# Top-32 attention with a gated product: weight splits evenly over stages 0 to 8, the sign of tile 1 on ScalarE from the first unit, the keys' low part later on GpSimd

## The chip, the cores and the metric

One core of a Trainium2 chip. The metric is the device time of one execution in microseconds, the median of three runs; the profile is of one further execution, whose own time is given beside its span.

## What is computed

```python
scores = scale * np.matmul(q, k.transpose(0, 1, 3, 2))       # q, k, v: 4 x 8 heads x 576 x 64
kth = np.partition(scores, -32, axis=-1)[..., -32:-31]
scores = np.where(scores >= kth, scores, -1e9)
attn = exp(scores - max) / (sum + 1e-9)
x = (attn @ v) as 2304 tokens x 512
out = ((x @ w_a) * (x @ w_b)) @ w_out                        # w_a, w_b: 512 x 1536, w_out: 1536 x 512
```

All is float32. The kernel multiplies in a faster format (fp32r) and keeps the accuracy by splitting each operand into a high part, which is the number rounded to that format, and a low part, which is what is left; each product is high x high + high x low + low x high.

## The kernel before, in words

A **unit** is a tile of 128 query rows for a pair of heads; there are 72, and a unit holds two tiles of scores (j = 0 and 1, one a head), 128 x 576 each. The order of units runs over the four batches. In **stage** s each engine does its share of a software pipeline whose order is written out by hand, in five loops over s from 0 to 78, one an engine; engines meet only in semaphores.

- VectorE works on unit s: four rounds of MAX8 (`find`) with MATCH_REPLACE8 between them (`take_out`), which give the 32 largest of each row; the inverse of unit s - 1's sums (`invert`) between the second round and the third; and at the end `below` (L1008), one compare a tile, which writes a large negative number to `keep` wherever a score is under the 32nd. From unit SIGN0 = 10 on only tile 0 has a compare. For tile 1 ScalarE computes the sign of (score - 32nd) into the top byte of `keep` (`mask_sign`, L715), over a fill value that VectorE's memset put there once.
- GpSimd, stage s: `negate(s-1)` (L882), which waits for VectorE's unit s - 1; the two masking adds `masked` (L901); `split_k`, the low part of keys that were prepared in stage s - 1 (L866); `hidden_lo`, the low part of a*b (L917); weight splits 2, 3, 4 of stage s - 1 (L856); `hidden`, the product a*b (L908); the low parts of x (L893) and q (L874); weight splits 0 and 1 of stage s.
- ScalarE, stage s: both exponentials of unit s - 1 (L724), `guard` (L732), split 0, `x_out`, the copy of b (L773), scores of the first half of unit s + 1 (L702), split 1, `normalise` of tile 0 (L739), scores of the second half, split 2, `normalise` of tile 1, the copies of the transposed probabilities (L747, L749), `mask_sign(s)`, `copy_q(s+3)`, split 3, the hidden copies (L780, L782), the copy of a, prepared keys, split 4.
- TensorE, stage s: probabilities times v of unit s - 2 (L557), scores of unit s + 1 (L523), the first product x @ w_a of chunk n = s - 5 (L588), turning a*b (L599), transposing the probabilities of unit s - 1 (L539), which waits for `normalise`, q's transposes (L501), the output product of chunk n - 2 (L620), and x @ w_b of chunk n.
- SP issues nearly all DMAs, in the same order of stages, and waits in it.

**Weights.** The 36 blocks of 128 x 512 come through a ring of four tiles `stage`. Block i is loaded by SP once the low part of block i - 4 is made; ScalarE rounds it into `w_hi` (L662); GpSimd subtracts (L856) into `w_lo`, or, for the 18 blocks whose low parts don't stay in SBUF (those of w_out and of w_b's last two row blocks, k 2 and 3), into one of LOWS buffers in the last slot of the ring of keys, from where SP stores it to scratch memory (L398) and reloads it per chunk. A low buffer is written again only when its store has landed. `W_ORDER` is the order of blocks, `W_AT` gives the (stage, place) of each split, with the places 0 to 4 named above; `columns_of` and `output` on TensorE wait for as many low parts as their first use needs. The order before is, for each third of the columns, eight blocks of w_a and w_b and then blocks of w_out (3, 3 and 6). `copy_k` of the slot that the low buffers share waits for all stores.

Of the kernel before, what the change touches and what calls it, by code (L numbers as in the profile page):

```python
# [6 lines left out]
def topk_attention_gated_product(nc, q, k, v, w_parts, xs, out):  # L7
# [8 lines left out]
    NEG = -3.0e38  # L16
# [4 lines left out]
    NF = DFF // P  # L21
# [6 lines left out]
    PAIR = 2 * S  # L28
# [8 lines left out]
    HB = HC // P  # L37
    NH = DFF // HC
    NCH = GROUPS * NH
# [50 lines left out]
    def preps_at(s):  # L90
        return [n for n in range(NPREPS) if PREP_SLOT[n] == s]


    SIGN0 = 10

    V_AT = {max(0, p - 1): [(0, p)] for p in range(1, KB)}
    V_AT[0] = [(0, 0), (0, 1)]
# [16 lines left out]
    for cb in range(NCB):  # L114
        W_BASE.append(len(W_ORDER))
        W_ORDER += [WB0 + kb * NCB + cb for kb in range(LKB, KB)] + [kb * NCB + cb for kb in range(KB)]
        W_ORDER += [WB0 + kb * NCB + cb for kb in range(LKB)]
        last = NF if cb == NCB - 1 else (cb + 1) * HB
        W_ORDER += [WO0 + f for f in range(cb * HB, last)]
    STAGES = 4  # L120
    W_AT = [(0, 2), (0, 4)] + [(1, m) for m in (0, 1, 2, 4)] + [(s, m) for s in range(2, 5) for m in range(5)]
    W_AT += [(s, m) for s in range(5, 9) for m in (0, 1, 2, 4)]
    W_AT = W_AT[:WCH]
    LOWS = 2
    LAST_IN_AB = NCH - NH - 1
    LATE_WO = (NCH - 4, NCH - 3, NCH - 2)
    LATE_WB = (NCH - 3, NCH - 1)

    def w_of(s, m):
        return [W_AT.index((s, m))] if (s, m) in W_AT else []  # L130


    LEAVING = [i for i in range(WCH) if W_ORDER[i] >= LOW]
# [5 lines left out]
    with ExitStack() as ctx:  # L139
# [37 lines left out]


        keys = k_t[:].rearrange("p k i c -> p (k i c)")
        leaving = keys[:, (KPAIRS - 1) * PAIR:(KPAIRS - 1) * PAIR + LOWS * WC].rearrange("p (n c) -> p n c", n=LOWS)  # L180

# [124 lines left out]
        def unit(u):  # L308
            return 0 <= u < NU
# [347 lines left out]
        def _(act):  # L657
# [6 lines left out]
            def weights(s, m):  # L664
                for i in w_of(s, m):
                    split_hi(i)

            def copy_k(n):
                act.wait_ge(kt_done, n + 1)
                if n >= KB - 1:  # L670
                    act.wait_ge(qt_done, min(PREP_SLOT[n] + 4, NU))
                if n >= KPAIRS:
                    wait(act, qk_done, 2 * last_unit((n - KPAIRS) // KB, (n - KPAIRS) % KB) + 2)
                elif n == KPAIRS - 1:
                    for m in range(LOWS):
                        act.wait_ge(st_w[m], 16 * len(range(m, len(LEAVING), LOWS)))
                for frm, a, z in keys_in_psum(n):
                    A.copy(k_t[:, n % KPAIRS, 0, a:z], frm[:, 0:z - a]).then_inc(khi_ready, 1)
                if n > 0:
                    wait(act, klo_ready, n - 1)  # L680
                    for frm, a, z in keys_in_psum(n):
                        last = A.copy(k_whole[:, a:z], frm[:, 0:z - a])  # L682
                    last.then_inc(k_copied, 1)
# [22 lines left out]
                A.copy(scores[:, 0, j, :].rearrange("p (a c) -> p a c", a=2), ps[:, j:j + 3:2, 0:HALF]).then_inc(s_ready, 1)  # L706

            def mask_sign(u):
                if not unit(u) or u < SIGN0:
                    return  # L710
                act.wait_ge(neg_ready, u + 1)
                if u == SIGN0:
                    act.wait_ge(s_keep, 1)
                act.wait_ge(mask_done, 2 * (u - 1) + 2)
                A.activation(keep_sign, scores[:, u % ROWS, 1, 0:S], ACT.Sign, bias=neg[:, u % 2, 1, 1:2], scale=SCALE  # L715
                             ).then_inc(keep_ready[1], 1)

# [86 lines left out]
            for s in range(FIRST, MOE_END):  # L804
# [18 lines left out]
                weights(s, 1)  # L823
                normalise(s - 1, 0)
                copy_scores(s + 1, 1)
                weights(s, 2)
                normalise(s - 1, 1)
                copy_probs_t(s - 1, 0)
                copy_probs_t(s - 1, 1)
                mask_sign(s)  # L830
                copy_q(s + 3)
                weights(s, 3)
                copy_hidden(n - 1)
# [2 lines left out]
                for m in preps_at(s):  # L836
                    copy_k(m)
                weights(s, 4)
                if s == NU + 1:
                    copy_y(n - 2)  # L840
            copy_y(NCH - 1)
# [2 lines left out]
        def _(pool):  # L844
# [81 lines left out]
            for s in range(FIRST, MOE_END):  # L926
                n = s - MOE0
                negate(s - 1)
                masked(s - 1, 0)
                masked(s - 1, 1)  # L930
                for m in preps_at(s - 1):
                    if m >= KB - 1:
                        split_k(m)
                if s < NU + 2 or n >= NCH:
                    hidden_lo(n - 2)
                for m in range(2, 5):
                    weights(s - 1, m)
                hidden(n - 1)
                low_of_x(s - 2)
                if s >= NU + 2 and n < NCH:  # L940
                    hidden_lo(n - 2)
                split_q(s + 2)
                weights(s, 0)
                weights(s, 1)

        @block.vector
        def _(dve):
# [15 lines left out]
            for h in range(2):  # L963
                rows = slice((1 - h) * TAIL, (2 - h) * TAIL)
                ins = V.memset(v_rows[rows, :, TAILS, h * D:(h + 1) * D], 0.0)
            ins.then_inc(s_vpad, 1)

            def find(u, r):
                nonlocal count
# [42 lines left out]
            for s in range(NU):  # L1012
# [11 lines left out]
                take_out(s, 2, 1)  # L1024
                find(s, 3)
                below(s, 0)
                if s < SIGN0:
                    below(s, 1)
                elif s == SIGN0:
                    dve.wait_ge(mask_done, 2 * s)  # L1030
                    V.memset(keep[:, 1, :], NEG).then_inc(s_keep, 1)
            invert(NU - 1)

# [28 lines left out]
```

## Time and profile before

| | us |
|---|---|
| median of 3 runs | 818.16 (817.97 to 818.72) |
| the profiled execution's own time | 817.8 |
| its span | 815.4 |
| PE, DVE, ACT, POOL busy | 771.7, 744.3, 657.0, 507.4 |
| granted TensorE clock, mean | 0.98 |

Lines with an L are lines of the kernel before. A timeline row is start, length, engine, line, operation, output<-inputs, shapes and count, and in brackets how long the engine stood idle before it and what ended that. Length of "x2" rows is that of both together. A wait row is: who waited, for whom, in total, how many times, the longest. All times are microseconds from the span's start.

### The profile page before, as it was taken

The numbers are of one execution on the slowest core, as the hardware profiler recorded it, in microseconds if no ns is written. First come the engines' busy times: TensorE is split into PE (matmuls) and PEld (weight loads), VectorE is DVE, ScalarE is ACT, GpSimd is POOL, SyncE is SP. The second block draws the span as 40 slices with busy tenths as digits, with TensorE's granted clock in tenths as the row PEclk, the third lists the DMA queues.
The fourth block names the chain that finished last, engine by engine and source line by source line (L and its number), as shares of the span: only waits on it lengthen the run. The fifth ranks groups of instructions, "written<-read, shape, count | busy, mean of one in ns | idle before, by whom it ended". The sixth has DMA issues, their size and how long they took to land.

```text
span 815.4 us, 18431 instructions
## 1 busy us (share of the span) xinstructions
PE 771.7 (95%) x5952; PEld 686.3 (84%) x5952; DVE 744.3 (91%) x1603; ACT 657.0 (81%) x1614; POOL 507.4 (62%) x560
## 2 busy tenths in 40 slices
PE   5368899999999999999999999999999999999998
PEld 4246788899998989898889899989998889898887
DVE  6999999998999999999999999999999999999500
ACT  5678978888888888888888888888888888888732
POOL 2989986656555666666756565665656555665532
PEclk9957999999999999999999999999999999999999
DMA  6566754445553444444644443544463434343562
GB/s 169 150 186 199 217 185 148 138 137 150 149 167 113 140 125 129 126 138 142 178 142 134 128 137 122 145 136 136 137 183 123 137 124 137 124 133 117 167 214 84
DMA packets 117245, 119.16 MB, mean 146 GB/s; under 512 B 61856, under 2 KB 80288, under 8 KB 117152
## 3 DMA queue, kind: packets, MB, share of 16 engines
q1 hardware_dynamic: 116880, 117.93, 47.8%
q8 instruction: 50, 0.82, 0.4%
q14 instruction: 43, 0.35, 0.2%
q10 hardware_dynamic: 272, 0.07, 0.0%
HBM read 108.53 MB, written 9.44 MB: 145 GB/s over the span
## 4 chain that ended last, share of the span: by engine, by line
PE 86%; POOL 5%; DVE 4%; DMA 2%; issue 2%; ACT 1%; SPq 0%; POOLq 0%; ACTq 0%
PE ps L588 37%; PE ps L620 18%; PE ps L557 10%; PE ps L523 9%; PE ps L539 8%; PE ps L599 3%; DVE best L976 2%; DVE work L993 2%; POOL scores L901 2%; POOL w_lo L856 1%; POOL k_t L856 1%; DMA x_scratch<-k_t 1%; PE ps L492 1%; PE ps L501 1%; DMA stage<-in_w 0%
## 5 line engine op out<-in xcount | busy, mean ns | idle before, releaser
L976 DVE MAX8 best<-work 128x8 f32<-128x576 f32 x432 | 304.4, 747 | 0.0
L901 POOL TENSOR_TENSOR scores<-scores,keep 128x576 f32<-128x576 f32 x144 | 207.0, 1441 | 37.4 <-ACT keep L715 36.6
L993 DVE MATCH_REPLACE8 work<-best,work 128x576 f32<-128x576 f32 x288 | 212.0, 745 | 0.0
L588 PE MATMUL ps<-w_hi,x_hi 128*128 128x384 f32 x576 | 202.5, 351 | 2.4 <-issue 1.2
L588 PE MATMUL ps<-w_hi,x_lo 128*128 128x384 f32 x576 | 194.4, 338 | 0.0
L908 POOL TENSOR_TENSOR ab<-ab 128x384 f32<-128x384 f32 x72 | 73.3, 1018 | 158.6 <-ACT ab L773 158.6
L588 PE MATMUL ps<-w_lo,x_hi 128*128 128x384 f32 x432 | 145.8, 337 | 0.0
L747 ACT COPY probs_t<-ps 128x512 f32<-128x512 f32 x144 | 82.2, 586 | 51.8 <-PE ps L539 49.7
L588 PEld LDWEIGHTS ps<-w_hi,x_hi 128*128 128x128 f32 x576 | 108.1, 188 | 17.5 <-issue 13.9
L724 ACT ACTIVATE scores<-scores,neg 128x576 f32<-128x576 f32 x144 | 114.4, 822 | 6.6 <-POOL scores L901 6.4
L739 ACT ACTIVATE scores<-scores,inverse 128x576 f32<-128x576 f32 x144 | 115.4, 803 | 0.3 <-DVE inverse L1003 0.3
L539 PE MATMUL ps<-ident,scores 128*128 128x128 f32 x648 | 90.1, 283 | 26.2 <-ACT scores L702 19.2
L588 PEld LDWEIGHTS ps<-w_hi,x_lo 128*128 128x128 f32 x576 | 108.1, 188 | 0.0
L993 DVE MATCH_REPLACE8 work<-best,scores 128x576 f32<-128x576 f32 x144 | 106.0, 745 | 0.0
L976 DVE MAX8 best<-scores 128x8 f32<-128x576 f32 x144 | 101.9, 750 | 2.5 <-ACT scores L706 2.5
L539 PEld LDWEIGHTS ps<-ident,scores 128*128 128x128 f32 x648 | 74.7, 145 | 33.5 <-ACT scores L739 17.8
L557 PE MATMUL ps<-probs_t,v_rows 128*64 128x128 f32 (+1 forms) x1600 | 99.5, 274 | 2.5 <-ACT probs_t L749 2.5
L557 PEld LDWEIGHTS ps<-probs_t,v_rows 128*64 128x64 f32 x1600 | 82.3, 141 | 21.0 <-issue 16.9
L702 ACT COPY scores<-ps 128x576 f32<-128x576 f32 x142 | 93.4, 658 | 2.0 <-PE ps L523 1.9
L620 PE MATMUL ps<-w_hi,h_hi 128*128 128x512 f32 x216 | 91.1, 422 | 0.5 <-issue 0.4
L523 PE MATMUL ps<-k_t,q_t 64*128 64x288 f32 x960 | 87.6, 319 | 3.3 <-ACT k_whole L682 1.9
L588 PEld LDWEIGHTS ps<-w_lo,x_hi 128*128 128x128 f32 x432 | 81.3, 188 | 3.0
(64 smaller groups left out, 1300.9 us busy)
## 6 DMA issues: line engine op xcount, KB each, us to landing
wo_lo<-x_scratch SPq DMA_DIRECT2D x69, 768.0 KB, 4.5
wb_lo<-x_scratch SPq DMA_DIRECT2D x70, 384.0 KB, 4.1
stage<-in_w SPq DMA_DIRECT2D x36, 256.0 KB, 3.1
x_scratch<-k_t SPq DMA_DIRECT2D x18, 256.0 KB, 2.4
k_rows<-in_k SPq DMA_DIRECT2D x32, 128.0 KB, 4.7
v_rows<-in_v SPq DMA_DIRECT2D x32, 128.0 KB, 2.6
out<-stage SPq DMA_DIRECT2D x16, 256.0 KB, 4.2
q_rows<-in_q SPq DMA_DIRECT2D x63, 64.0 KB, 3.5
```

Source lines behind the costliest of these rows:

```text
L523: last = mm(ps_s[half][:, j, :], q_t[rows, u % 2, qpart, first:first + 2 * D], k_t[rows, (b * KB + p) % KPAIRS, kpart, at:at + HALF], star ...
L539: last = tr(to, row_of(u)[:, at:at + P], ident[:])
L557: last = mm(ps_x[h * D:(h + 1) * D, i * w:(i + 1) * w], v_rows[:, p, block, h * D:(h + 1) * D], probs_t[:, at:at + w], start=(i == 0 and c ...
L588: last = mm(ps_ab[which], x[:, g % 2, kb, :], w, start=(kb == 0 and m == 0), stop=(kb == KB - 1 and m == 2))
L620: last = mm(ps_y, x[:, cols], w, start=(f + b == 0 and m == 0), stop=(f + b == NF - 1 and m == 2))
L702: A.copy(scores[:, u % ROWS, :, half * HALF:(half + 1) * HALF], ps_s[half]).then_inc(s_ready, 1)
L724: A.activation(row, row, ACT.Exp, bias=neg[:, u % 2, j, 0:1], scale=SCALE, accum_out=sums[:, u % 2, j:j + 1]).then_inc(e_ready, 1)
L739: A.mul(row, row, inverse[:, u % 2, j:j + 1]).then_inc(p_ready, 1)
L747: A.copy(probs_t[:, a:a + FULL * P], ps[:, 2 + j, :]).then_inc(pt_ready, 1)
L901: V.tensor_tensor(row, row, keep[:, j, :], ALU.add).then_inc(mask_done, 1)
L976: ins = V.max(best[:, u % 2, j, 8 * r:8 * r + 8], src)
L993: V.match_replace(out=work[:, j, :], in_to_replace=best[:, u % 2, j, 8 * r:8 * r + 8], in_values=src, imm_value=NEG).then_inc(chain, 1)
```

## The change

It does three things:

1. Weights: all blocks of w_out come last in `W_ORDER`. `W_AT` has four splits a stage in stages 0 to 2, five in 3 to 5, three in 6 to 8 (before: 2, 4, 5, 5, 5, 4, 4, 4, 3). There are four low buffers (LOWS) in place of two, over the last two slots of the ring of keys, so the wait for all stores stands at the preparation of the fifth pair of keys (n = 4, stage 10) instead of the sixth (stage 12).
2. `mask_sign` runs for all units. In stages 0 and 1 it stands at the end of ScalarE's stage, from stage 2 on behind the copies of the transposed probabilities. VectorE's second compare is gone, its memset of the fill value stands before its first unit.
3. On ScalarE `normalise` of tile 1 stands before weight split 2 instead of behind it; on GpSimd `split_k` stands behind `hidden_lo`.

```diff
-    SIGN0 = 10
+    SIGN_LATE = 1
...
-        last = NF if cb == NCB - 1 else (cb + 1) * HB
-        W_ORDER += [WO0 + f for f in range(cb * HB, last)]
+    W_ORDER += [WO0 + f for f in range(NF)]
     STAGES = 4
-    W_AT = [(0, 2), (0, 4)] + [(1, m) for m in (0, 1, 2, 4)] + [(s, m) for s in range(2, 5) for m in range(5)]
-    W_AT += [(s, m) for s in range(5, 9) for m in (0, 1, 2, 4)]
-    W_AT = W_AT[:WCH]
-    LOWS = 2
+    W_AT = [(s, m) for s in range(3) for m in (0, 1, 2, 4)] + [(s, m) for s in range(3, 6) for m in range(5)]
+    W_AT += [(s, m) for s in range(6, 9) for m in (0, 1, 2)]
+    LOWS = 4
...
-        leaving = keys[:, (KPAIRS - 1) * PAIR:(KPAIRS - 1) * PAIR + LOWS * WC].rearrange("p (n c) -> p n c", n=LOWS)
+        leaving = keys[:, (KPAIRS - 2) * PAIR:(KPAIRS - 2) * PAIR + LOWS * WC].rearrange("p (n c) -> p n c", n=LOWS)
...
-                elif n == KPAIRS - 1:
+                elif n == KPAIRS - 2:
...
             def mask_sign(u):
-                if not unit(u) or u < SIGN0:
+                if not unit(u):
                     return
                 act.wait_ge(neg_ready, u + 1)
-                if u == SIGN0:
+                if u == 0:
                     act.wait_ge(s_keep, 1)
-                act.wait_ge(mask_done, 2 * (u - 1) + 2)
+                wait(act, mask_done, 2 * (u - 1) + 2)
...
                 copy_scores(s + 1, 1)
+                normalise(s - 1, 1)
                 weights(s, 2)
-                normalise(s - 1, 1)
                 copy_probs_t(s - 1, 0)
                 copy_probs_t(s - 1, 1)
-                mask_sign(s)
+                if s > SIGN_LATE:
+                    mask_sign(s)
...
                 weights(s, 4)
+                if s <= SIGN_LATE:
+                    mask_sign(s)
...
                 masked(s - 1, 1)
+                if s < NU + 2 or n >= NCH:
+                    hidden_lo(n - 2)
                 for m in preps_at(s - 1):
                     if m >= KB - 1:
                         split_k(m)
-                if s < NU + 2 or n >= NCH:
-                    hidden_lo(n - 2)
...
             ins.then_inc(s_vpad, 1)
+            V.memset(keep[:, 1, :], NEG).then_inc(s_keep, 1)
...
                 below(s, 0)
-                if s < SIGN0:
-                    below(s, 1)
-                elif s == SIGN0:
-                    dve.wait_ge(mask_done, 2 * s)
-                    V.memset(keep[:, 1, :], NEG).then_inc(s_keep, 1)
```

## Rows read from the trace of the kernel before

**Rows 1.** The page: busy time by engine; busy tenths of GpSimd, slices of 20.4 us.

```profile
PE 771.7 (95%) x5952; PEld 686.3 (84%) x5952; DVE 744.3 (91%) x1603; ACT 657.0 (81%) x1614; POOL 507.4 (62%) x560
...
POOL 2989986656555666666756565665656555665532
```

**Rows 2.** Waits, 108 to 765 us: who, for whom, total us, times, longest.

```profile
DVE inverse L1003 <- ACT sums_eps L732: 14.2, 15, 1.8
...
PE ps L539 <- ACT scores L739: 1.4, 1, 1.4
```

**Rows 3.** The chain that ended last, 0 to 125 us: start, length, what.

```profile
102.42 0.34 SPq L398
...
102.80 3.56 DMA stage<-in_w
...
106.91 0.78 ACT scores L739
```

**Rows 4.** Timeline of ScalarE, 9 to 112 us, then 443 to 466 us.

```profile
57.68 0.20 ACT L732 ACTIVATE sums_eps<-sums 128x2 f32<-128x2 f32 x1
...
60.57 0.62 ACT L662 CAST w_hi<-stage 128x512 fp32r<-128x512 f32 x1 [1.30 <-DMA stage<-in_w]
...
65.48 0.27 ACT L749 COPY probs_t<-ps 128x128 f32<-128x128 f32 x1
...
68.68 0.20 ACT L732 ACTIVATE sums_eps<-sums 128x2 f32<-128x2 f32 x1
...
106.38 0.62 ACT L662 CAST w_hi<-stage 128x512 fp32r<-128x512 f32 x1 [1.00 <-DMA stage<-in_w]
...
444.73 0.97 ACT L715 ACTIVATE keep<-scores,neg 128x576 int8<-128x576 f32 x1
```

**Rows 5.** Timeline of TensorE, 60 to 125 us.

```profile
86.28 0.41 PE L588 MATMUL ps<-w_hi,x_hi 128*128 128x384 f32 x1 [0.78 <-issue]
...
95.93 0.76 PE L539 MATMUL ps<-ident,scores 128*128 128x128 f32 x5 [1.44 <-ACT scores L739]
...
107.73 0.77 PE L539 MATMUL ps<-ident,scores 128*128 128x128 f32 x5 [1.42 <-ACT scores L739]
...
112.73 1.31 PE L557 MATMUL ps<-probs_t,v_rows 128*64 128x128 f32 x20
```

**Rows 6.** Timeline of VectorE, 0 to 120 us, then 443 to 466 us.

```profile
10.29 1.42 DVE L976 MAX8 best<-scores 128x8 f32<-128x576 f32 x2 [2.48 <-ACT scores L706]
...
51.63 0.94 DVE L1008 TENSOR_SCALAR keep<-scores,best 128x576 f32<-128x576 f32 x2
...
62.19 1.97 DVE L1008 TENSOR_SCALAR keep<-scores,best 128x576 f32<-128x576 f32 x2
...
97.41 1.41 DVE L976 MAX8 best<-scores 128x8 f32<-128x576 f32 x2
...
443.87 1.43 DVE L976 MAX8 best<-scores 128x8 f32<-128x576 f32 x2
...
449.42 0.17 DVE L1003 RECIPROCAL inverse<-sums_eps 128x2 f32<-128x2 f32 x1
...
454.00 1.43 DVE L976 MAX8 best<-scores 128x8 f32<-128x576 f32 x2
```

**Rows 7.** Timeline of GpSimd, 70 to 125 us, then 443 to 466 us.

```profile
96.70 0.44 POOL L882 TENSOR_SCALAR neg<-best 128x4 f32<-128x4 f32 x1
...
101.12 2.51 POOL L856 TENSOR_TENSOR k_t<-stage,w_hi 128x512 fp32r<-128x512 f32 x2
...
443.64 0.41 POOL L882 TENSOR_SCALAR neg<-best 128x4 f32<-128x4 f32 x1 [1.33 <-DVE best L976]
```

**Rows 8.** Line 856: what GpSimd idled for before it, us and times.

```profile
  DMA x_scratch<-k_t: 3.0, 5
```

**Rows 9.** Windows: length, busy PE, PEld, DVE, ACT, POOL, PEclk, DMA, GB/s.

```profile
65.00:70.00 5.00, 4.37 (x34) 3.59 (x33) 5.00 (x13) 4.97 (x15) 5.00 (x5) 0.50 0.33 97
70.00:75.00 5.00, 3.27 (x20) 2.74 (x21) 5.00 (x9) 3.85 (x7) 4.13 (x6) 0.98 0.86 267
```

More of the change, by code:

```diff
@@ L129, in w_of @@
     def w_of(s, m):
-        return [W_AT.index((s, m))] if (s, m) in W_AT else []
+        return [i for i in range(WCH) if W_AT[i] == (s, m)]
     LEAVING = [i for i in range(WCH) if W_ORDER[i] >= LOW]
```

## The prediction

> **What bounds the kernel now.** I read the page first: TensorE is busy 771.7 us of 815.4 and VectorE 744.3, so either could set the end [rows 1]. Next, who waited from 108 to 765 us: TensorE for another engine only once, 1.4 us, and that is the wait that ends at 107.73, the beginning of this stretch [rows 2]. After 107.73 the end is therefore TensorE's own work in a fixed order, which the change leaves alone, and VectorE's waits there, 14.2 us in 15 times [rows 2], cost nothing. So the kernel is 107.7 us of filling and about 708 us of TensorE with hardly a pause; the change is worth what it moves TensorE's last wait.
>
> The chain of waits up to there [rows 3]: SP stores a low part at 102.42 and behind that loads the next block, 3.56 us. ScalarE has stood 1.00 us at this split and takes it at 106.38 [rows 4]; only then does it scale tile 1 of unit 7 (106.91, done 107.68 by 0.77 of work). TensorE has waited 1.42 us for that, and 1.44 us for the same thing a stage earlier, at 95.93 [rows 5]. From 107.73 it has 5.0 us to the product with v that opens its next stage at 112.73 [rows 5].
>
> Beneath this lies VectorE's pace. I call start(s) the time at which it begins unit s: start(0) = 10.29, start(8) = 97.41, so a unit takes 10.89 in the mean; in the steady part 454.00 - 443.87 = 10.13 [rows 6]. Two things make the difference. Units 0 to 9 have a second compare (L1008). And where GpSimd is busy at a unit's end the pair of compares takes 1.97 us in place of 0.94 [rows 6]; so it is in three of the eight units, and in a fourth by half.
>
> The sum needs start(8) and the distance from it to the end of the last scaling of unit 7.
>
> **Part 1: sign of tile 1 on ScalarE from unit 0.** Ten compares go, and one sign comes in each of units 0 to 9: 0.97 us on ScalarE, as later on [rows 4]. The fill value's memset (a pass over one tile, about half of the pair's 0.94) moves ahead of VectorE's first search, where it idles 2.48 for scores [rows 6]: nothing. Eight units at 10.13 from 10.29 put start(8) at 91.3, against 97.41.
>
> That is too good by the port. In units 4 to 7 the one remaining compare still finds GpSimd in a run of subtractions, 2.51 for two [rows 7]. The bounds are 0 (all slip in between two) and 1.0 each, as 1.97 - 0.94; I take the half, 0.5 x 4 = **2.0**, bounds 0 to 4.0. The Trainium skill (SBUF — State Buffer, "SBUF: two separate sides") has VectorE and GpSimd hold a shared port pair as an exclusive lock for a whole instruction. The trace agrees (1.97 for 0.94); by that rule every compare that comes second pays the rest of a subtraction; with all four paying 1.0 the time would be 2.0 us later than mine.
>
> The new wait: GpSimd's second masking add now waits for ScalarE. Queued behind it on GpSimd are the weight splits, the product a*b and the low parts of x and q, for which SP's next loads and ScalarE's next splits wait. The sign itself stands, from unit 2 on, behind the copies of the transposed probabilities of the unit before; behind it come copy_q, splits 3 and 4, the hidden copies and both exponentials. That closes a loop. From the end of one guard (57.88) to the last of those copies (65.75) it is 7.9 us now, 1.30 of it a wait for a weight at 60.57; from there to the next guard's end (68.88) 3.1 [rows 4]; with the sign between, 0.85 of ScalarE's time as it overlaps its neighbour, 11.9 in all, over 10.13. Part 3 takes one split, 0.5, off the first piece; of the 1.30 I keep 0.9 in stages 4 and 5, which have five splits still, and 0 from stage 6 on. So some 11.2 there (a little more with the copy of a), 10.4 after. VectorE's play: the inverse stands 5.55 us into a unit (449.42 - 443.87, [rows 6]); a guard that nothing delays ends 4.4 into it (negation 0.23 before the start and 0.41 long, two adds 2.9, exponential and guard 1.2), so 1.1 us. Walked with these pieces: guard 3 ends at 56.1, needed at 50.8 + 5.55 = 56.4, just in time. Stage 4: 56.1 + 11.3 = 67.4 against, with one port wait, 61.4 + 5.55 = 67.0; 0.4 late. Stage 5: 67.4 + 11.2 = 78.6 against 72.4 + 5.55 = 78.0; 0.6 late. Sum **1.0**, bounds 0 and 3.0 (three stages 1 us late each).
>
> So start(8) = 91.3 + 2.0 + 1.0 = 94.3, between 91.3 and 98.3.
>
> **Part 2: weights.** The 36 splits and 18 stores stay; they stand 4, 4, 4, 5, 5, 5, 3, 3, 3 in stages 0 to 8, where they stood 2, 4, 5, 5, 5, 4, 4, 4, 3. GpSimd has two fewer of them between 20 and 104 us, 2.5 us. With the third product's last, columns of w_a and w_b are whole sooner: TensorE's wait of 0.78 before 86.28 [rows 5], ahead of x @ w_b, goes, but it then only stands longer at the scaling: 0 by itself. Needs stay met: the last low part, index 35, is split in stage 9 and used in stage 10. Four buffers in place of two take away GpSimd's waits for a store, 3.0 us in 5 times [rows 8]: a buffer comes up again after four splits, 5 us. If they stayed, VectorE's play would cover 1.1 of each. In stage 0 SP's queue now meets two stores and two loads around the loads of v and ahead of one of q; these slip some 4 us and are used after 30: nothing, and once 4 us if that cover were gone. Most of all, the last load is issued in stage 7 (before: behind stage 8's first wait, at 102.80), and stages 7 and 8 have three splits whose data were asked for a stage before: the 1.00 wait at 106.38 goes.
>
> **Part 3: order on ScalarE and GpSimd.** Scaling of tile 1 ahead of split 2: its 0.53 (106.91 - 106.38) leaves the path, and so does any wait before it. The keys' low part moves behind the low part of a*b, so it is an instruction of some 1.0 us later where keys are prepared, for keys needed three units on, nearly all of it behind 107.7 where TensorE waits for nobody: 0, bounds -0.5 to +0.5.
>
> **The sum.** From start(8) to the scaling's end is now 107.68 - 97.41 = 10.3. It loses 1.00 + 0.53. It gains 0.5: the negation starts 0.71 before the next unit now (96.70 against 97.41) because two compares stand in between, and 0.23 in the steady part (443.64 against 443.87, [rows 6, 7]). So 9.2, and the scaling ends at 94.3 + 9.2 = 103.5 in place of 107.7: 4.2 us sooner. TensorE is there in time: released for unit 6 at about 93.3 it needs 5.0 to its stage's opening and 4.7 to the next such transposes, 103.0. The profiled execution took 817.8 (span 815.4), 0.4 below the median of the runs; 817.8 - 4.2 = 813.6, and on the median **814.0**.
>
> **Rivals.**
> *A, VectorE's pace whole.* No port waits and no late inverse: start(8) = 91.3, scaling done at 100.5, 7.2 us sooner, 811.0. For it: three of the eight units have a 0.94 pair although GpSimd works; against: GpSimd stays nine tenths busy over these slices [rows 1]. Chance 0.12.
> *B, GpSimd keeps the bound.* The splits are only shuffled, each compare comes second (4.0) and the loop costs 2.0: start(8) = 97.3, scaling 106.5, 1.2 sooner, 817.0. For it: GpSimd's total falls by only 2.5 us in 84. The port rule of the Trainium skill (as above) leads here. Chance 0.18.
> *C, slower: the ring through ScalarE.* If the load waits stay as they are, the loop is 11.9 in stages 2 to 8 against 11.0 a unit now: 0.9 x 6 = 5.4 more, less the 1.1 that the last stage wins by itself: 4.3 later, 822.5. It decides once the last copy of the probabilities ends over 1.6 us after the negation. Against: four loads in flight keep their distance, and the worst waits lie in splits that move. Chance 0.08.
> *D, TensorE's clock.* It was granted 0.50, the 1.2 GHz level, up to 70 us and 0.98 after, behind a stretch busy 4.37 of 5 [rows 9]. If it came back a stage later, one stage's 7 us of work would take 14, with 3 of slack: 4 us, which eats the gain, 818.2. Chance 0.05.
> *E, nothing moves*, because something else releases TensorE at 107: 0.02.
>
> **How the numbers follow.** The forecast has 0.55; its own bounds (0 to 4.0, 0 to 3.0) give 811.0 to 818.0, both ends only if both terms are extreme together. From 811.0 to 817.2 takes in A and B and leaves out C, D, E and a little at each end, 0.2. The measurement tells 0.2% apart, 1.6 us: faster means under 816.5. Faster: forecast 0.53, A 0.12, B 0.08, 0.73. Same: B 0.10, D 0.03, E 0.02, forecast 0.02, 0.17. Slower: C 0.08, D 0.02, 0.10.
>
> **What would show it.** One L1008 a unit from unit 0, start(8) near 94.3, inverse waits of about half a microsecond in units 5 and 6; GpSimd adds that wait for a sign, 1 us or less, in stages 2 and 4 to 6; no weight wait before the scalings of units 6 and 7; TensorE's last wait before 105 and 708 us from there to the end as now. Wrong, if TensorE waits for a scaling beyond 108, if its clock is at half beyond 72, or if the stretch behind its last wait changes.

## The result and the profile after

| | before | after |
|---|---|---|
| median, same chip | 818.07 us (4 runs, 817.77 to 818.72) | 810.45 us (4 runs, 810.32 to 810.86) |
| the profiled execution's own time | 817.8 | 810.42 |
| its span | 815.4 | 808.3 |

The ratio is 0.9907, with a 95% interval of 0.989 to 0.9924: 7.6 us faster, where 4.2 were forecast, and 0.55 below the range. Medians and ratios in this document leave out one disturbed execution each of e8, e10 and g1 (4191, 1887 and 1255 us), and e10's profile is of that one.

Busy time, to be held against [rows 1]: VectorE lost 5.7 us and ten instructions, ScalarE gained 6.5 and ten, and GpSimd, as full as before up to 100 us, has a 7 for an 8 in the slice behind it.

```profile
PE 769.5 (95%) x5952; PEld 688.5 (85%) x5952; DVE 738.6 (91%) x1593; ACT 663.5 (82%) x1624; POOL 505.4 (63%) x560
...
POOL 3999976666555666666655666666655565655532
```

TensorE's timeline of after, the rows that answer to [rows 5]. The transposes for which it stood 1.42 us at 107.73 now begin, in one row with those of tile 0, at 102.94 without a wait that the profile shows; the last such wait ends at 92.57. The scaling of tile 1 of unit 7 ends at 103.37, and stage 9 opens 5.05 behind it at 108.42, as before (107.68 and 112.73), so that scaling still sets the opening.

```profile
82.50 1.35 PE L537 MATMUL ps<-ident,scores 128*128 128x128 f32 x9 [1.16 <-ACT scores L700]
...
85.02 0.42 PE L586 MATMUL ps<-w_hi,x_hi 128*128 128x384 f32 x1 [1.06 <-issue]
...
92.57 1.35 PE L537 MATMUL ps<-ident,scores 128*128 128x128 f32 x9 [0.33 <-ACT scores L700]
...
102.94 1.25 PE L537 MATMUL ps<-ident,scores 128*128 128x128 f32 x9
...
108.42 1.31 PE L555 MATMUL ps<-probs_t,v_rows 128*64 128x128 f32 x20
...
139.44 1.31 PE L555 MATMUL ps<-probs_t,v_rows 128*64 128x128 f32 x20
```

VectorE's timeline of after, beside [rows 6]: one L1010 (before L1008) a unit, start(0) = 10.24, start(8) = 93.64. Two of the compares ran into GpSimd, 1.44 and 1.35 for some 0.52, and one inverse came late, by 0.38.

```profile
10.24 1.42 DVE L978 MAX8 best<-scores 128x8 f32<-128x576 f32 x2 [1.75 <-ACT scores L704]
...
70.60 1.44 DVE L1010 TENSOR_SCALAR keep<-scores,best 128x576 f32<-128x576 f32 x1
...
81.70 1.35 DVE L1010 TENSOR_SCALAR keep<-scores,best 128x576 f32<-128x576 f32 x1
...
88.98 0.17 DVE L1005 RECIPROCAL inverse<-sums_eps 128x2 f32<-128x2 f32 x1 [0.38 <-ACT sums_eps L730]
...
93.14 0.57 DVE L1010 TENSOR_SCALAR keep<-scores,best 128x576 f32<-128x576 f32 x1
...
93.64 1.41 DVE L978 MAX8 best<-scores 128x8 f32<-128x576 f32 x2
...
124.23 1.44 DVE L978 MAX8 best<-scores 128x8 f32<-128x576 f32 x2
```

I add up both kernels by TensorE's openings, the products with v (L555, before L557), one a stage:

| | before | after | gain |
|---|---|---|---|
| stage 9 opens | 112.73 | 108.42 | 4.31 |
| stage 9 and 10 together | 20.87 | 20.87 | 0 |
| stage 11 | 11.04 | 10.15 | 0.89 |
| stage 12 opens | 144.64 | 139.44 | 5.20 |
| stages 13, 29, 33, 49, together | 42.44 | 40.69 | 1.75 |
| all other time from stage 12 to the end | 628.35 | 628.17 | 0.18 |
| span | 815.43 | 808.30 | 7.13 |

So the filling up to stage 9 gave what was forecast. Two gains lie behind 107.7, where the forecast had none: 0.9 in stage 11 and 1.8 in four stages spread over the steady part. The experiments are on these two, and on which part of the change earned the 4.3.

### The profile page after: what moved, and what is told of

Read it like the earlier page. It is cut to its first block, busy times and chain, and to the rows that moved or that the text cites. A ratio compares the mean times of both kernels' runs of the same rounds, so it can differ in the third digit from the quotient of the medians.

```text
span 808.3 us, 18438 instructions
## 1 busy us (share of the span) xinstructions
PE 769.5 (95%) x5952; PEld 688.5 (85%) x5952; DVE 738.6 (91%) x1593; ACT 663.5 (82%) x1624; POOL 505.4 (63%) x560
## 4 chain that ended last, share of the span: by engine, by line
PE 89%; DVE 5%; POOL 2%; issue 2%; ACT 1%; DMA 1%; SPq 0%; POOLq 0%; ACTq 0%
PE ps L586 38%; PE ps L618 19%; PE ps L555 10%; PE ps L521 9%; PE ps L537 8%; PE ps L597 3%; DVE best L978 2%; DVE work L995 2%; PE ps L490 1%; DMA stage<-in_w 1%; PE ps L499 1%; POOL w_lo L857 1%; POOL scores L902 1%; POOL k_t L857 0%; DMA k_rows<-in_k 0%
## 5 line engine op out<-in xcount | busy, mean ns | idle before, releaser
L978 DVE MAX8 best<-work 128x8 f32<-128x576 f32 x432 | 308.4, 766 | 0.0
L995 DVE MATCH_REPLACE8 work<-best,work 128x576 f32<-128x576 f32 x288 | 214.9, 766 | 0.0
L586 PE MATMUL ps<-w_hi,x_hi 128*128 128x384 f32 x576 | 202.7, 352 | 2.0 <-issue 1.1
L586 PE MATMUL ps<-w_hi,x_lo 128*128 128x384 f32 x576 | 194.6, 338 | 0.0
L586 PE MATMUL ps<-w_lo,x_hi 128*128 128x384 f32 x432 | 146.1, 338 | 0.0
L586 PEld LDWEIGHTS ps<-w_hi,x_hi 128*128 128x128 f32 x576 | 108.4, 188 | 16.7 <-issue 13.7
L586 PEld LDWEIGHTS ps<-w_hi,x_lo 128*128 128x128 f32 x576 | 108.4, 188 | 0.0
L555 PE MATMUL ps<-probs_t,v_rows 128*64 128x128 f32 (+1 forms) x1600 | 99.4, 274 | 2.5 <-ACT probs_t L747 2.5
L555 PEld LDWEIGHTS ps<-probs_t,v_rows 128*64 128x64 f32 x1600 | 82.2, 141 | 21.0 <-issue 16.8
L586 PEld LDWEIGHTS ps<-w_lo,x_hi 128*128 128x128 f32 x432 | 81.6, 189 | 3.0
```

The source lines that it names most:

```text
L555: last = mm(ps_x[h * D:(h + 1) * D, i * w:(i + 1) * w], v_rows[:, p, block, h * D:(h + 1) * D], probs_t[:, at:at + w], start=(i == 0 and c ...
L586: last = mm(ps_ab[which], x[:, g % 2, kb, :], w, start=(kb == 0 and m == 0), stop=(kb == KB - 1 and m == 2))
L978: ins = V.max(best[:, u % 2, j, 8 * r:8 * r + 8], src)
L995: V.match_replace(out=work[:, j, :], in_to_replace=best[:, u % 2, j, 8 * r:8 * r + 8], in_values=src, imm_value=NEG).then_inc(chain, 1)
```

## The experiments

Each line is against the kernel before on the same chip. The last four columns are from the profiled execution: start(8), start(11) of VectorE, and the openings of TensorE's stages 9 and 12 (there is no row for e10_norm_alone; h2_norm_again is the same kernel). The ratio is made round by round and can stand a little off that of the medians. "Rest" is from the opening of stage 12 to the end of the span.

| kernel | us against before | ratio (95%) | start(8) | start(11) | stage 9 | stage 12 | rest |
|---|---|---|---|---|---|---|---|
| before | | | 97.41 | 130.30 | 112.73 | 144.64 | 670.79 |
| after | -7.6 | 0.9907 (0.989 to 0.9924) | 93.64 | 124.23 | 108.42 | 139.44 | 668.86 |
| e1_splitk_alone | -1.4 | 0.998 (0.9971 to 0.9988) | 98.05 | 130.93 | 115.17 | 146.20 | 668.92 |
| e2_splitk_back | -5.4 | 0.9933 (0.992 to 0.9945) | 94.21 | 126.05 | 110.20 | 141.21 | 670.77 |
| e6_before_own_h | -2.2 | 0.9971 (0.996 to 0.9982) | 97.83 | 130.62 | 112.97 | 144.76 | 668.85 |
| e7_after_own_h | -7.8 | 0.9904 (0.9892 to 0.9917) | 92.91 | 123.54 | 107.70 | 138.71 | 668.71 |
| e8_sign_alone | +1.2 | 1.0014 (1.0005 to 1.0024) | 98.86 | 131.73 | 116.39 | 147.39 | 670.50 |
| e9_weights_alone | -0.9 | 0.9993 (0.9984 to 1.0002) | 96.06 | 130.50 | 112.78 | 144.86 | 670.69 |
| h2_norm_again | -0.1 | 0.9999 (0.999 to 1.0007) | 97.52 | 130.40 | 110.64 | 144.77 | 670.72 |
| h1_norm_weights | -2.8 | 0.9964 (0.9952 to 0.9977) | 96.54 | 128.41 | 109.66 | 142.75 | 670.41 |
| e3_norm_back | -2.2 | 0.9976 (0.9967 to 0.9985) | 98.04 | 130.28 | 114.94 | 145.94 | 668.60 |
| e4_weights_back | -5.5 | 0.9937 (0.9923 to 0.995) | 95.74 | 127.13 | 111.04 | 142.07 | 668.95 |
| e5_sign_back | -5.3 | 0.9934 (0.9921 to 0.9946) | 95.63 | 127.50 | 108.76 | 141.65 | 668.63 |
| f1_early_splits | -9.4 | 0.9883 (0.9869 to 0.9897) | 92.67 | 123.33 | 106.33 | 137.50 | 669.02 |
| g1_scale_first | -7.9 | 0.99 (0.9885 to 0.9914) | 93.79 | 124.41 | 108.40 | 139.41 | 668.89 |
| k1_early_own_h | -9.3 | 0.9887 (0.9874 to 0.9901) | 93.12 | 123.73 | 106.72 | 137.93 | 668.84 |
| k2_early_first | -8.9 | 0.9892 (0.9877 to 0.9907) | 93.13 | 124.21 | 107.18 | 138.41 | 668.70 |

### The 1.8 us in the steady part: the keys' low part

**e1_splitk_alone**: the kernel before, with only the move on GpSimd.

```diff
                 masked(s - 1, 1)
+                if s < NU + 2 or n >= NCH:
+                    hidden_lo(n - 2)
                 for m in preps_at(s - 1):
                     if m >= KB - 1:
                         split_k(m)
-                if s < NU + 2 or n >= NCH:
-                    hidden_lo(n - 2)
```

> The kernel before with one edit: on GpSimd the keys' low part behind the low part of a*b. The changed kernel was 7.6 us faster (4.3 of it by the opening of stage 9), and 2.65 us of the rest lie in five later TensorE stages (11, 13, 29, 33, 49), each shorter by 0.42 to 0.90. Theory K: this edit makes them shorter, because ScalarE's copy of b waits for the low part of a*b and all of ScalarE's stage stands behind it: this kernel is 2.2 to 2.8 us faster than before, about 815.5, and TensorE's filling up to stage 9 is unchanged within 0.3. Theory S: the five stages are shorter because the switch to the sign at unit 10 is gone and the phase between the engines is another: this kernel is within 0.5 us of before.

Measured: rest 668.92 in place of 670.79, the whole of the gain behind stage 12. The median falls by 1.4. Its profiled execution hides that: it was the slowest of this kernel, 817.68, and in it TensorE's clock fell to half at 108.5 to 112, of which more at the end.

**e2_splitk_back**: the kernel after, with those lines in the old order again.

> The changed kernel with the keys' low part put back ahead of the low part of a*b. Theory K: 2.2 to 2.8 us slower than the changed kernel, about 813.1 (5.0 faster than before). Theory S: as the changed kernel, 810.5.

Measured: rest 670.77, as before; 2.2 us of the 7.6 are lost.

What does it do? Here is stage 13 of the kernel before in three timelines, GpSimd, ScalarE and TensorE. Keys are split first, then comes the low part of a*b (L917), and ScalarE's copy of b (L773) stands 0.34 for that, because it writes over the tile which L917 reads. Behind the copy of b stand both copies of scores (L702) and both scalings, and TensorE's transposes (L539) wait for them.

```profile
154.97 1.42 POOL L866 TENSOR_TENSOR k_t<-k_whole,k_t 128x576 fp32r<-128x576 f32 x1 [1.24 <-ACT k_whole L682]
156.35 1.01 POOL L917 TENSOR_TENSOR h_lo<-ab,h_hi 128x384 fp32r<-128x384 f32 x1
```

```profile
157.47 0.48 ACT L773 COPY ab<-ps 128x384 f32<-128x384 f32 x1 [0.34 <-POOL h_lo L917]
```

```profile
155.34 1.31 PE L557 MATMUL ps<-probs_t,v_rows 128*64 128x128 f32 x20
...
159.25 0.49 PE L599 MATMUL ps<-ident,ab 128*128 128x128 f32 x3
159.84 1.35 PE L539 MATMUL ps<-ident,scores 128*128 128x128 f32 x9
161.02 0.27 PE L501 MATMUL ps<-ident,q_rows 128*128 128x128 f32 x1
...
165.94 1.31 PE L557 MATMUL ps<-probs_t,v_rows 128*64 128x128 f32 x20
```

The same stage of after, ScalarE and then TensorE:

```profile
151.82 0.50 ACT L771 COPY ab<-ps 128x384 f32<-128x384 f32 x1
```

```profile
150.14 1.31 PE L555 MATMUL ps<-probs_t,v_rows 128*64 128x128 f32 x20
...
154.05 0.49 PE L597 MATMUL ps<-ident,ab 128*128 128x128 f32 x3
154.38 1.17 PE L537 MATMUL ps<-ident,scores 128*128 128x128 f32 x9
155.39 0.27 PE L499 MATMUL ps<-ident,q_rows 128*128 128x128 f32 x1
...
160.31 1.31 PE L555 MATMUL ps<-probs_t,v_rows 128*64 128x128 f32 x20
```

Count from the stage's opening: the copy of b begins at 2.13 before and 1.68 after; TensorE turns a*b at 3.91 in both; the transposes begin at 4.50 and 4.24, those of q at 5.68 and 5.25, and the stage takes 10.60 and 10.17. So TensorE stood some 0.4 us, in two steps: the transposes of tile 0 also wait for the second copy of scores, done at 159.70, and those of tile 1 for its scaling, done at 160.36. Its matmul rows name no wait: the turning ends at 159.74 by its modelled end and the transposes begin at 159.84, 0.10 later. Its weight-load rows (PEld) of the same stage name both:

```profile
159.81 0.42 PEld L539 LDWEIGHTS ps<-ident,scores 128*128 128x128 f32 x4 [0.30 <-issue]
160.42 0.53 PEld L539 LDWEIGHTS ps<-ident,scores 128*128 128x128 f32 x5 [0.19 <-ACT scores L739]
```

In after the nine weight loads of this stage (154.27) are one row without a wait. So the waits of before in the stretch 108 to 765 us, the list that the prediction went by, had it twice, on TensorE's weight loads and on ScalarE:

```profile
ACT ab L773 <- POOL h_lo L917: 2.7, 8, 0.3
PEld ps L539 <- issue: 2.2, 7, 0.3
...
PEld ps L539 <- ACT scores L739: 1.3, 7, 0.2
```

The seven of TensorE lie in stages 11, 13, 29, 33 and 49, the five that became shorter, and in 21 and 57. After keeps only the last two (100 to 758 us):

```profile
PEld ps L537 <- issue: 0.6, 2, 0.3
PEld ps L537 <- ACT scores L737: 0.4, 2, 0.2
```

Four of ScalarE's eight are the stages that became shorter. In the other four, such as the one at 189.72, TensorE computes 24 pieces of scores and not 12 (1.86 us, L523); its transposes come 5.05 or 5.6 behind the opening anyway, and the late copy is covered. Those stages have the same length in after.

The Trainium skill (Perfetto Trace Analysis, "Tensor Engine Instruction (MATMUL, LD_WEIGHTS)") says that TensorE's end times are computed from an instruction's size and not observed; this stage agrees: the turning begins 3.91 behind the opening in both kernels and the transposes 0.26 later in before, of which its matmul rows show 0.10. The rest of the 0.43 lies inside the row of nine, 1.35 long against 1.17.

**e6_before_own_h**: to tell the wait from the order. The kernel before in the old order of GpSimd, but the copy of the whole a*b goes to a tile of its own, so that the copy of b has nothing to wait for.

```diff
+        h_whole = sb("h_whole", [P, HC])
...
-            return ab[:, 1, :] if n < LAST_IN_AB else keep[:, 0, 0:HC]
+            return h_whole[:] if n < LAST_IN_AB else keep[:, 0, 0:HC]
...
-                    wait(act, h_lo_ready, min(n, LAST_IN_AB))
```

> The kernel before, where the transposed a*b gets a tile of its own (h_whole) and no longer shares ab's second half with b, so that the copy of b waits for no low part; order of work unchanged. Theory K: what costs is ScalarE's wait in the copy of b, so this gives the same 2.2 to 2.8 us as moving the keys' low part, about 815.5. If the gain came from the keys' low part being later or GpSimd's order in another way: within 0.5 us of before.

Measured: rest 668.85, 2.2 us faster; its stage 13 takes 10.17. The order by itself costs nothing; the wait of the copy of b was the cause, and the change's move is one of two ways to be rid of it.

**e7_after_own_h**: the same edit on the kernel after.

> The changed kernel with a tile of its own for the transposed a*b. In the kernel before this gave 2.2 us, as much as moving the keys' low part did. If both only take away ScalarE's wait for the low part of a*b, nothing is left here: within 0.5 us of the changed kernel, 810.0 to 811.0. If the tile had a use of its own: under 810.

Measured: rest 668.71; nothing is left to gain there. Its median, 810.05, is 0.4 under that of after, with ratios whose intervals overlap.

### The 0.9 us in stage 11: two limits, and the later one counts

**e10_norm_alone and h2_norm_again** are one kernel, the one before with the scaling of tile 1 ahead of split 2. It ran twice.

```diff
                 copy_scores(s + 1, 1)
+                normalise(s - 1, 1)
                 weights(s, 2)
-                normalise(s - 1, 1)
```

> The kernel before with one edit: on ScalarE the scaling of tile 1 ahead of weight split 2. In the changed kernel taking this edit back cost 5.3 us; the sign alone made the kernel before 1.2 slower. Theory R (ring): the edit is worth so much only where the sign stands behind the copies of the probabilities; here, where no sign follows in units 0 to 9, it takes 0.53 and the wait of 1.00 off the last scaling and no more: 1.0 to 2.0 us faster, 816 to 817. Theory T: earlier transposes help TensorE whatever the sign does: 3 us or more faster, 815 or less (the changed kernel without the sign is 5.3 faster than before, of which about 1.8 lie behind stage 9).

> The kernel before with the scaling of tile 1 ahead of split 2 alone, once more, for a trace of an undisturbed execution: 817.2 to 818.0. If the ring theory holds, the start of unit 8 stays at 97.4 within 0.5, the last scaling ends 1 to 1.5 earlier than 107.68, and the wait that the split at 106.38 had is found again on another instruction of ScalarE or on TensorE.

Measured: 0.9995 (0.9986 to 1.0004) and 0.9999, no change, where 1.0 to 2.0 us were expected of the first run. Yet stage 9 opens 2.09 us sooner. TensorE's timeline of h2_norm_again, and then VectorE's, show who takes it back:

```profile
104.83 0.52 PE L599 MATMUL ps<-ident,ab 128*128 128x128 f32 x3 [0.77 <-issue]
...
110.64 1.31 PE L557 MATMUL ps<-probs_t,v_rows 128*64 128x128 f32 x20
...
115.14 0.52 PE L599 MATMUL ps<-ident,ab 128*128 128x128 f32 x3 [0.43 <-issue]
...
116.28 1.35 PE L539 MATMUL ps<-ident,scores 128*128 128x128 f32 x9 [0.62 <-ACT scores L702]
...
144.77 1.31 PE L557 MATMUL ps<-probs_t,v_rows 128*64 128x128 f32 x20
```

```profile
130.40 1.35 DVE L976 MAX8 best<-scores 128x8 f32<-128x576 f32 x2
```

TensorE now has waits where it had none, and stage 12 opens at 144.77, as before (144.64), because VectorE begins unit 11 at 130.40, as before (130.30). From there to the opening of stage 12 it is 14.37 here, 14.34 in before. In VectorE's timeline of the kernel before the beginning of unit 11 is

```profile
129.83 0.54 DVE L1031 MEMSET keep<- 128x576 f32 x1
130.30 1.35 DVE L976 MAX8 best<-scores 128x8 f32<-128x576 f32 x2
```

so stage 12 stood on VectorE, with second compares in units 8 and 9 and the memset in unit 10 (that unit takes 10.74 in every kernel that has the memset there, 10.13 in the others). I had put the handover to TensorE at 107.7. The two limits, read from the table:

- TensorE's: opening of stage 12 = opening of stage 9 + 31.0. It holds in after, e1, e2, e3, e4, e7, e8 and g1 (31.00 to 31.03).
- VectorE's: opening of stage 12 = start(11) + 14.35, or + 14.15 where the copy of b has no wait. It holds in before (14.34), e9 (14.36), h1 (14.34), h2 (14.37), and in e5 (14.15), e6 (14.14), f1 (14.17), k1 (14.20) and k2 (14.20).

The later of the two gives the opening of stage 12 in all 17 profiles of the table to within 0.06 us; the constants were read from these same profiles, so this is a fit. The edits that bear it out are h2, which moves stage 9 and not start(11), and e5 below, which against after moves start(11) by 3.3 and stage 9 by only 0.3. Units 8 to 10 together, start(8) to start(11), take 32.89 in before, 31.87 in e5 and 30.59 in after. In before VectorE's is later (144.64 against 143.7), in after TensorE's (139.44 against 138.4): 0.9 of stage 11 went because both limits moved, TensorE's by 4.3 and VectorE's by 6.3. This wait too stood on TensorE's weight loads in the list above, in stage 11.

### Which part earns the filling

**e8_sign_alone**: the kernel before with ScalarE's sign for all units and the compares gone (and the memset of the fill value moved to the start), and nothing else.

```diff
-                if not unit(u) or u < SIGN0:
+                if not unit(u):
...
+                if s > SIGN_LATE:
+                    mask_sign(s)
...
+                if s <= SIGN_LATE:
+                    mask_sign(s)
...
-                if s < SIGN0:
-                    below(s, 1)
```

> The kernel before with the sign of tile 1 on ScalarE from unit 0 and nothing else (second compare gone, memset moved). By my sum: eight units at 10.13 put the start of unit 8 at 91.3, with 2.0 of port waits; the ring through ScalarE is 11.9 a stage with the old splits and the old place of the scaling, so it costs more than in the full change: 2 to 3 us. Start of unit 8 at 95.3 to 96.3, 815.9 to 817. Rival C as in the prediction: the ring takes over in stages 2 to 8, 820 to 822.5. From the run without the new weights (5.4 faster, of which 2.4 belong to the keys' move) sign and scaling together are worth 3.0: that would be 815 to 816 here.

Measured: 0.14% slower, where 1 to 2 us faster were expected. Waits from 0 to 112 us in its profile:

```profile
ACT w_hi L662 <- DMA stage<-in_w: 7.4, 7, 1.9
...
POOL scores L904 <- ACT keep L715: 6.1, 6, 2.5
...
DVE inverse L1007 <- ACT sums_eps L732: 4.7, 5, 1.3
```

This is rival C's ring: loads delay ScalarE's splits, these the scalings, the probabilities and the sign behind them, GpSimd's add waits for the sign, the exponentials and VectorE's inverse for the add. VectorE gets ten compares less and loses 4.7 at the inverses.

**e3_norm_back**: the kernel after, with split 2 ahead of the scaling of tile 1 again.

> The changed kernel with the scaling of tile 1 behind weight split 2 again. My sum: 0.53 on the path of the last scaling, and in stages 4 to 6 another 0.5 a stage of the ring, of which VectorE's play takes part: 0.5 to 1.5 us slower than the changed kernel, 811.0 to 812.0. Since TensorE's last wait there is now 0.33 in stage 7 and nothing in stage 8, it could also be 0.

Measured: 5.4 of the 7.6 are lost, where 0.5 to 1.5 were expected: the dearest part to leave out, though it is worth nothing alone. From 0 to 112 us, with e3's adds on GpSimd for the sign in the first row:

```profile
POOL scores L902 <- ACT keep L713: 7.5, 6, 2.0
...
DVE inverse L1005 <- ACT sums_eps L730: 3.7, 5, 1.6
```

In after these are 2.0 in three times and 0.38 once:

```profile
POOL scores L902 <- ACT keep L713: 2.0, 3, 1.0
```

The scaling ahead of split 2 takes one wait for a load out of the ring (ScalarE's waits for loads are 4.9 us in 5 times in e3, 3.5 in 4 in after); sign and scaling pay together. No run has these two alone. e4 has them with the keys' move and gives 5.5, and the keys' move gives 1.4 by e1 and 2.2 by e2, so I estimate the two at 3.3 to 4.1 together, where each alone gave nothing or less.

**e9_weights_alone**: the kernel before with the new W_ORDER, W_AT and LOWS. **h1_norm_weights**: that and the scaling's move. **e4_weights_back**: after with the old weights. **e5_sign_back**: after with the old sign and compares.

> The kernel before with the weights' part alone: order of blocks, even places, four low buffers. Theory V (VectorE's pace bounds the filling, the last load's wait of 1.0 comes on top): 1.0 to 1.5 us faster, about 817. Theory G (GpSimd bounds it): 2.4 us faster as in the other direction, where taking the new weights out cost 2.35, about 815.8.

> The kernel before with the weights' part and the scaling of tile 1 ahead of split 2; no sign in units 0 to 9, keys' low part as before. Alone the weights gave 0.9 and the scaling 0.1. Theory P (pairs): each takes away what hides the other: together with the keys' move they gave 5.3, and the keys give 1.4 to 2.4, so about 3 to 3.9 here: 814.0 to 815.2. Theory A (they add): 1.0, about 817, and the keys' move is worth more in that company.

> The changed kernel with the weights as before (order of blocks, places of the splits, two low buffers), so before plus the sign from unit 0 and both moves. My sum gave the weights the 1.0 us wait at the last scaling and let GpSimd's two splits fewer go for play: with the 2.7 us of the keys' move that makes about 812.5, 2 us slower than the changed kernel. Rival: the weights carry the filling's gain, since GpSimd is nine tenths busy there and the sign alone only adds a ring through ScalarE: 814.5 to 816.

> The changed kernel with the second compare back on VectorE in units 0 to 9. Theory V: VectorE loses 0.42 in eight units and its second wait for the port in some: 3.4 to 6 us slower than the changed kernel, 814 to 816. Theory G: the compares fill time in which GpSimd is behind anyway: under 2 us slower, 812.5.

Measured: weights alone -0.9, an interval that just takes in no change; weights and scaling -2.8; and to leave one out of the full change costs 2.1 (weights) and 2.3 (sign). Alone the four parts (-1.4, +1.2, -0.9, -0.1) add up to -1.2; by what each costs when left out (2.2, 5.4, 2.1, 2.3), to 12.0; the change gives 7.6. So only the keys' move has a worth that hardly depends on the rest. e5 shows why best: its stage 9 opens at 108.76, hardly later than in after, but its start(11) is 127.50 for 124.23, so VectorE's limit gives 141.65.

### Is more to be had

**f1_early_splits**: GpSimd was still full in stages 3 to 6 of after, so stage 0 gets six splits, two each at its first two places, in place of four.

```diff
-    W_AT = [(s, m) for s in range(3) for m in (0, 1, 2, 4)] + [(s, m) for s in range(3, 6) for m in range(5)]
-    W_AT += [(s, m) for s in range(6, 9) for m in (0, 1, 2)]
+    W_AT = [(0, 0), (0, 0), (0, 1), (0, 1), (0, 2), (0, 4)] + [(s, m) for s in range(1, 7) for m in (0, 1, 2, 4)]
+    W_AT += [(s, m) for s in (7, 8) for m in (0, 1, 2)]
```

> The changed kernel with six splits in stage 0 (two each at places 0 and 1), four in stages 1 to 6 and three in 7 and 8. GpSimd idled about 4 us before its first negation, so four low parts fit there and stages 3 to 5 lose one each. If GpSimd's load in stages 3 to 6 sets the filling: 1 to 2.5 us faster than the changed kernel, 808 to 809.5. If the ring through ScalarE does, whose place 1 waits for a load in those stages as before: within 0.7 of it.

Measured: 808.54 us, 1.9 below after, the best of all. In VectorE's timeline all inverses come in time and the dear compares are 0.73, 0.78 and 1.34, where after had 1.44 and 1.35. That makes start(8) 0.97 sooner; stage 9 is 2.09 sooner, since the scaling of unit 7 ends 8.6 behind start(8) where it took 9.7. The last two of these compares:

```profile
80.99 0.78 DVE L1010 TENSOR_SCALAR keep<-scores,best 128x576 f32<-128x576 f32 x1
...
91.41 1.34 DVE L1010 TENSOR_SCALAR keep<-scores,best 128x576 f32<-128x576 f32 x1
```

**g1_scale_first**: after with both scalings ahead of splits 1 and 2, to see whether the loads that ScalarE still waits for (3.5 us in 4 times up to 108 us) cost anything.

```diff
-                weights(s, 1)
                 normalise(s - 1, 0)
                 copy_scores(s + 1, 1)
                 normalise(s - 1, 1)
+                weights(s, 1)
                 weights(s, 2)
```

> The changed kernel with both scalings ahead of weight splits 1 and 2 on ScalarE. Ring theory: the waits for a weight at place 1 (1.15, 1.04 and 0.89 in stages 4 to 6) and the splits' 0.53 leave the ring between guard and sign; TensorE's waits of 2.03, 1.16, 1.06 and 0.33 in stages 5 to 7 shrink by about half: 1 to 2.5 us faster than the changed kernel, 808 to 809.5. Rival: split 1 an instruction later makes its low part and the next load later, so GpSimd loses what ScalarE wins: 810 to 811.5.

Measured: as after within the intervals, where 1 to 2.5 us were expected. TensorE's waits at 82.50 and 92.57 are gone, and a longer one stands at L586, 2.66 where after had 1.06 at 85.02, so that start(8) and stage 9 are where they were:

```profile
84.33 0.41 PE L586 MATMUL ps<-w_hi,x_hi 128*128 128x384 f32 x1 [2.66 <-issue]
```

**k1_early_own_h** is f1 with e7's tile, **k2_early_first** is f1 with g1's order.

> The changed kernel with six splits in stage 0 (which gave 1.9 us over the changed kernel) and the transposed a*b in a tile of its own (0.4 there). Filling theory: the two act in different places, so they add: 807.8 to 808.4. If not: 808.5 as with the six splits alone.

> Six splits in stage 0 and both scalings ahead of splits 1 and 2. The latter alone gave 0 in the median: in its trace the sum of waits for weights only moved from places 1 to places 2 to 4. With the earlier splits those waits are gone from stages 4 to 6, so only 0.53 of split 1 a stage is left to win: 807.5 to 808.5; if TensorE's own waits for low parts (0.5 to 0.8 at L586) bound stages 5 to 7 now: 808.5 to 809.5.

Measured: 808.86 and 809.20, neither better than f1. All three now stand on VectorE's limit of stage 12 (14.17 to 14.20 behind start(11)) with TensorE's 0.2 us ahead of it, so a sooner stage 9 alone can give nothing more.

## Why the prediction was wrong

**What held.** The sum up to the last scaling of unit 7: start(8) 93.64 (forecast 94.3), scaling done 103.37 (103.5), opening of stage 9 sooner by 4.31 (4.2). The port term, 2.0, was measured at 1.96: eight compares took 6.12 in all, 8 x 0.52 = 4.16 without GpSimd. It came in another shape, two whole and six free instead of four halves. By the port rule of the Trainium skill (SBUF — State Buffer, "SBUF: two separate sides") a compare that comes second pays the rest of a subtraction; these two paid about 0.9 each, so the trace agrees, but most compares did not come second. The loop's term, 1.0, was 0.38: once late, in stage 7, where the walk had two. The distance from start(8) to the scaling's end was 9.73 and not 9.2, and start(8) came 0.66 sooner than forecast, so two errors of some half a microsecond cancel, by luck. Adds that wait for the sign: 2.0 us in three times, none over 1.0, as said. The last wait of TensorE before a transpose came before 105, as said. One reading was wrong and the sum did not use it: of the eight pairs of compares in before, two (62.19 and 73.79) pay the whole port wait and one (95.97, 1.52) half, not three and one; the pair of 1.95 at 107.12 is unit 8's.

**The step that failed** is the first one: "After 107.73 the end is therefore TensorE's own work in a fixed order", and with it the check "708 us from there to the end as now" and Part 3's "where TensorE waits for nobody: 0". It failed twice.

1. *Part 3, the keys' move, put at 0 (bounds -0.5 to +0.5), gave 1.8.* I read the rows of TensorE's matmuls in the list of waits and took a missing entry for no wait. Those rows work with modelled ends, and in stage 13 they left 0.10 us, too little for the list. The wait stood in the same list twice: on the weight loads before the transposes, seven times, and one engine up, as the 2.7 us that ScalarE's copy of b waits for GpSimd, eight times. So "TensorE for another engine only once" was a misreading. I had asked only who needs the keys, and not who waits for what stood behind the keys on GpSimd. e1, e2 and e6 show it.
2. *The handover, put at 107.7, was later, worth 0.9.* VectorE's waits were rightly seen as harmless, but VectorE itself was not yet ahead: in units 8, 9 and 10 it had the second compares and the memset, and stage 12 stood on it (start(11) + 14.35). The compares of these units left with the change and were priced at nothing. h2, which wins 2.09 at stage 9 and none at the end, and e5, which puts the compares back and opens stage 9 only 0.34 later but stage 12 2.21 later, show it, and the two limits fit all 17 kernels.

With these, 4.2 + 1.8 + 0.9 = 6.9, which would have given 810.9 for the profiled execution; it took 810.42.

**The rivals.** A (811.0) is nearest in number, by luck, and wrong in mechanism: two compares did wait for the port, and start(8) is 93.64 and not 91.3. B did not come: its two terms of 4.0 and 2.0 were 1.96 and 0.38. C, the ring, is real: e8 is slower by it, with inverses late by 4.7. It was turned off by the scaling's move and the weights, as the forecast had it, but in e3 it takes back 5.4. I had it right that the waits for loads decide, and had put the scaling's move at only 0.53 and the wait before it; its larger effect is inside the ring. D: the clock was at half once beyond 72, up to 74, so that sign of being wrong did come, and it was back at full from 74; the sum for start(8), 8 x 10.13 + 1.96 + 0.38 = 83.4, which is 93.64 - 10.24, leaves no room for a price of it there, and the distance from the last scaling to stage 9 is 5.05 as before. E did not come.

## What to carry to other kernels

- Where TensorE's work is said to run without a pause, read the waits of its weight loads (PEld) too, and compare the lengths of its equal stages: four of 10.6 among others of 10.17 were a wait that its matmul rows did not have and its weight-load rows did. The engine one step up shows it as well.
- A filling ends at the later of two limits, and a gain on one is given back until the other moves; find both as "event plus constant" before pricing an edit, and expect edits on a ring to be worth little alone and much together.

## What the runs showed of the hardware

**TensorE's clock differs between executions.** Its mean over e1's eleven executions of one kernel went from 0.964 to 1.0. In the profiled executions the granted clock stood at the lower level (0.50, 1.2 GHz) from 39.5 to 70 us in before, from 46.5 to 67 and 70.5 to 74 in after, and in e1, after three such stretches up to 78, once more from 108.5 to 112, behind a stretch in which TensorE was busy 1.32 of 3.5 us. Windows of after and then of e1; columns are the stretch, its length, busy PE, PEld, DVE, ACT, POOL, the granted clock, DMA share, GB/s:

```profile
72.00:74.00 2.00, 2.00 (x9) 1.82 (x8) 2.00 (x5) 1.52 (x4) 1.52 (x2) 0.51 0.77 207
74.00:78.00 4.00, 4.00 (x42) 3.58 (x43) 4.00 (x11) 3.97 (x12) 3.49 (x3) 1.00 0.10 29
```

```profile
105.00:108.50 3.50, 1.32 (x11) 0.95 (x9) 3.50 (x9) 1.73 (x4) 2.83 (x5) 1.00 0.92 280
108.50:112.00 3.50, 3.44 (x11) 2.98 (x12) 3.50 (x7) 2.57 (x10) 3.50 (x4) 0.52 0.45 152
```

e1's stage 8, in which that stretch falls, took 14.26, 11.79 in before. Its stage 12 opens at 146.20 by TensorE's limit, where VectorE's gives 145.1, so I estimate the price in this execution at 1.1 us; it took 817.68, 0.8 above its kernel's median. That this is the spread of the other executions is not shown: the mean clock does not order them (816.17 us at 0.968, 817.15 at 0.981). After's executions lie within 0.54 us, so the clock is no explanation for the 7.6. What decides where the stretches fall was not tried.
